# An attention and two feed-forward layers on one core: GpSimd takes the next weight slot's sums first, ScalarE splits weights a step sooner and the product first

## The reference

```python
kv  = einsum('bhsd,bhse->bhde', k, v)            # B=4, H=8, S=576, D=64
out = einsum('bhsd,bhde->bhse', q, kv)
x   = out / sqrt(mean(out**2, -1) + 1e-6) * g_norm    # then (2304, 512)
g   = x @ w_gate; val = x @ w_val                     # 512 -> 1536
x   = (g * sigmoid(g) * val) @ w_out                  # 1536 -> 512
h   = x @ w_in                                        # 512 -> 2048
y   = softplus(h) @ w_out2                            # 2048 -> 512
```

## Time and profile before

| what | value |
|---|---|
| median of 3 runs | 890.45 us |
| the profiled execution | 890.55 us, of it span 888.8 us |
| PE | busy 877.7 us, 99% of the span |
| PEld (weight loads) | 814.4 us, 92% |
| DVE | 645.2 us, 73% |
| ACT | 441.5 us, 50% |
| POOL | 229.7 us, 26% |
| granted clock of TensorE | 1.0 in all 40 slices |

### The profile page before, as it was taken

The page is one execution under the profiler, slowest core; times in us unless marked ns, Lnnn a source line. Parts: engine busy times, 40 slices in busy tenths (PEclk is TensorE's granted clock), DMA queues, the critical chain, the costliest instruction groups (busy, mean ns, idle before and its releaser), DMA issues.

```text
span 888.8 us, 14699 instructions
## 1 busy us (share of the span) xinstructions
PE 877.7 (99%) x5362; PEld 814.4 (92%) x5362; DVE 645.2 (73%) x1254; ACT 441.5 (50%) x778; POOL 229.7 (26%) x189
## 2 busy tenths in 40 slices
PE   8999999999899999999999999999999999999998
PEld 7999999999899999999999999999999999999997
DVE  3555665777575866676777998878878878878875
ACT  4617464664342544343345664554554554554553
POOL 4644203289820398730255000000000000000000
PEclk9999999999999999999999999999999999999999
DMA  9985865442200022010034110000000000000100
GB/s 270 227 213 151 154 139 127 126 114 72 72 1 1 1 72 68 22 44 1 1 96 129 62 48 0 36 0 0 35 0 0 35 0 0 35 0 0 37 1 36
DMA packets 95541, 53.93 MB, mean 61 GB/s; under 512 B 37248, under 2 KB 86528, under 8 KB 95488
## 3 DMA queue, kind: packets, MB, share of 16 engines
q1 hardware_dynamic: 95328, 53.23, 22.5%
q10 hardware_dynamic: 160, 0.00, 0.0%
HBM read 44.96 MB, written 8.26 MB: 60 GB/s over the span
## 4 chain that ended last, share of the span: by engine, by line
PE 88%; POOL 5%; DVE 2%; issue 2%; ACT 1%; DMA 1%; SPq 1%; DVEq 0%; ACTq 0%; POOLq 0%
PE bank L951 20%; PE bank L953 20%; PE bank L952 20%; PE bank L1110 7%; PE bank L1109 7%; PE bank L1108 7%; POOL slots L748 2%; PE bank L891 1%; PE bank L884 1%; POOL slots L751 1%; PE bank L959 1%; POOL slots L743 1%; DMA raw_out<-in_moe_w_out 0%; POOL slots_sums L734 0%; POOL slots_sums L732 0%
## 5 line engine op out<-in xcount | busy, mean ns | idle before, releaser
L951 PE MATMUL bank<-x_hi,arena 128*128 128x384 f32 x554 | 187.0, 338 | 0.0
L953 PE MATMUL bank<-x_hi,arena 128*128 128x384 f32 x554 | 186.8, 337 | 0.0
L952 PE MATMUL bank<-x_lo,arena 128*128 128x384 f32 x554 | 186.0, 336 | 0.0
L951 PE MATMUL bank<-ring,slots 128*128 128x256 f32 x504 | 143.1, 284 | 3.4 <-DVE sum_b L1595 2.5
L952 PE MATMUL bank<-ring,slots 128*128 128x256 f32 x504 | 142.6, 283 | 0.0
L953 PE MATMUL bank<-ring,slots 128*128 128x256 f32 x504 | 142.6, 283 | 0.0
L1333 ACT ACTIVATE act_a<-bank 128x384 f32<-128x384 f32 x96 | 47.2, 491 | 173.9 <-PE bank L953 173.9
L1110 PE MATMUL bank<-arena,g_lo 128*128 128x512 f32 x288 | 113.1, 393 | 0.0
L1109 PE MATMUL bank<-arena,g_hi 128*128 128x512 f32 x288 | 112.9, 392 | 0.0
L1108 PE MATMUL bank<-arena,g_hi 128*128 128x512 f32 x288 | 111.9, 388 | 0.0
L951 PEld LDWEIGHTS bank<-x_hi,arena 128*128 128x128 f32 x554 | 104.4, 188 | 4.0
(11 more groups left out here) (140 smaller groups left out, 1653.5 us busy)
## 6 DMA issues: line engine op xcount, KB each, us to landing
stage<-in_moe_w_out SPq DMA_DIRECT2D x28, 256.0 KB, 3.8
out_dram<-out_stage SPq DMA_DIRECT2D x18, 256.0 KB, 2.1
k<-in_k SPq DMA_DIRECT2D x16, 256.0 KB, 3.3
v<-in_v SPq DMA_DIRECT2D x16, 256.0 KB, 3.2
stage<-in_moe_w_in SPq DMA_DIRECT2D x16, 256.0 KB, 2.8
xy<-in_q SPq DMA_DIRECT2D x48, 72.0 KB, 3.0
stage<-in_moe_w_gate SPq DMA_DIRECT2D x12, 256.0 KB, 3.8
stage<-in_moe_w_val SPq DMA_DIRECT2D x12, 256.0 KB, 4.0
```

The lines of the kernel that those rows point to most:

```text
L951: nc.tensor.matmul(ps, hi, rhs_hi, start=first, stop=False)
L952: nc.tensor.matmul(ps, hi, rhs_lo, start=False, stop=False)
L953: return nc.tensor.matmul(ps, lo, rhs_hi, start=False, stop=last)
```

## The change

`weight_highs(f)` now also makes the output's high part, so that part comes ahead of the sums' high part in the counts of `w7_hi_ready`, and `HIGH7_AT` and `SUM_HIGH7_AT` put slots 0 to 2 one step sooner (slot 8's raw high one later). On POOL the sums' low part becomes a function of its own, and the next slot's sums stand ahead of it; the output's low part stands ahead of both, and `load7_out` waits only for that. SP issues the loads of slot 2 and the w_out of slot 1 two tiles sooner. On ACT `g7_high(q)` stands ahead of `weight_sum_highs`.

```diff
-LOWS7_RAW = 2
+LOWS7_RAW, LOWS7_OUT = 2, 3
...
-HIGH7_AT = {19: 0, 20: 1, 22: 2, 25: 3, 26: 4, 27: 5, 38: 6, 39: 7, 40: 8, 42: 9, 43: 10, 44: 11}
+HIGH7_AT = {18: 0, 19: 1, 21: 2, 24: 3, 25: 4, 26: 5, 38: 6, 39: 7, 41: 8, 42: 9, 43: 10, 44: 11}
-SUM_HIGH7_AT = {20: 0, 21: 1, 24: 2, 25: 3, 26: 4, 27: 5, 38: 6, 39: 7, 41: 8, 42: 9, 43: 10, 45: 11}
+SUM_HIGH7_AT = {19: 0, 20: 1, 22: 2, 24: 3, 25: 4, 26: 5, 38: 6, 39: 7, 41: 8, 42: 9, 43: 10, 45: 11}
...
         def load7_out(f):
...
-                sp.wait_ge(w7_ready, LOWS7 * f)
+                sp.wait_ge(w7_ready, LOWS7 * (f - 1) + LOWS7_OUT)
...
         load7_up(1)
-        for j in range(1, NT - 1):
+        keep_x(3, 1)
+        fetch_x(3, 1)
+        load7_up(2)
+        load7_out(1)
+        for j in range(2, NT):
             keep_x(3, j)
             fetch_x(3, j)
-        load7_up(2)
-        load7_out(1)
-        keep_x(3, NT - 1)
-        fetch_x(3, NT - 1)
...
             pool.wait_ge(w7_hi_ready, 3 * f + 2)
+            nc.gpsimd.tensor_tensor(slots7[:, f % SEG, RAW7 + OUT7:SLOT7], raw7_out[:, :],
+                                    slots7[:, f % SEG, OUT7:RAW7].bitcast(F32), ALU.subtract).then_inc(w7_ready, 1)
+
+        def weight_sum_lows(f):
+
+            pool.wait_ge(w7_hi_ready, 3 * f + 3)
             for i in (3, 5):
                 nc.gpsimd.tensor_tensor(w7_part(f, 1, i, i + 2), w7_sum(f, i, i + 2),
                                         w7_part(f, 0, i, i + 2).bitcast(F32), ALU.subtract).then_inc(w7_ready, 1)
-            pool.wait_ge(w7_hi_ready, 3 * f + 3)
-            nc.gpsimd.tensor_tensor(slots7[:, f % SEG, RAW7 + OUT7:SLOT7], raw7_out[:, :],
-                                    slots7[:, f % SEG, OUT7:RAW7].bitcast(F32), ALU.subtract).then_inc(w7_ready, 1)
...
-        for f in range(SEG):
+        weight_sums(0)
+        weight_lows(0)
+        weight_sums(1)
+        weight_sum_lows(0)
+        weight_lows(1)
+        weight_sum_lows(1)
+        weight_sums(2)
+        weight_lows(2)
+        first_x_sum(1)
+        for f in range(3, SEG):
             weight_sums(f)
+            weight_sum_lows(f - 1)
             weight_lows(f)
-            if f == 1:
-                first_x_sum(1)
+        weight_sum_lows(SEG - 1)
...
         def weight_highs(f):
...
+            act.wait_ge(raw7_out_loaded, 16 * (f + 1))
+            nc.scalar.activation(slots7[:, f % SEG, OUT7:RAW7], raw7_out[:, :], ACT.Copy).then_inc(w7_hi_ready, 1)
 
         def weight_sum_highs(f):
...
-            act.wait_ge(raw7_out_loaded, 16 * (f + 1))
-            nc.scalar.activation(slots7[:, f % SEG, OUT7:RAW7], raw7_out[:, :], ACT.Copy).then_inc(w7_hi_ready, 1)
...
+            g7_high(q)
             if k in SUM_HIGH7_AT:
                 weight_sum_highs(SUM_HIGH7_AT[k])
-            g7_high(q)
```

More of the change, by code:

```diff
@@ L794, in _ @@
         first_x_sum(3)
-        for f in range(SEG, NF1):
+        weight_sums(SEG)
+        weight_lows(SEG)
+        for f in range(SEG + 1, NF1):
             weight_sums(f)
+            weight_sum_lows(f - 1)
             weight_lows(f)
+        weight_sum_lows(NF1 - 1)
         x_sums(3)
```

## The result

The changed kernel is slower by 0.7%: 897.19 us, the median of 6 runs (895.88 to 898.24), against 890.58 us for the kernel before (6 runs, 889.33 to 892.93). The ratio is 1.0072, with a 95% interval of 1.0055 to 1.0088. The forecast was 897.7. The profiled execution took 896.48 us with a span of 894.7; before it was 890.55 with 888.8. On ACT, VectorE and TensorE the lines of the changed kernel have numbers 16 higher than before, apart from the weight work itself (L1231 is now L1247, L1236 is L1254, L1238 is L1249).

What follows compares the result with a forecast made beforehand. TensorE, busy 99% of the span, was taken as the bound, so only its idle time counts. 0.4 + 8.15 + 2.5 + 0.1 - 3.9 = +7.25 us on 890.55, less 0.1, gave 897.7 us; range 893.0 to 901.0.

Steps and rivals of the forecast that it cites:

- Slot 2: Step 21: ACT waits for a w_out load queued behind work its own root starts; cost 8.15 us, bounds 5 and 10.
- VectorE's slow instruction: Ring's low part beside POOL's sums' lows of slot 1 takes 2.48 us, not 0.83; root late by 1.7 us.
- The clock: Behind slot 2's wait the granted clock falls; 5 us slow, 2.5 us lost, bounds 0 and 3.5.
- Slot 1: Step 19: w_out lands at 176.4, so silu(20) ends after TensorE wants up1(21); cost 0.4 us, bounds 0 and 1.5.
- The later slots: From seven-product step 0: late w_out landings stay covered; three ACT instructions ahead of sum_a expose 0.1 us, up to 1.5.
- The gain: Five TensorE waits at new weight slots vanish through the product's earlier place and POOL's earlier sums; 3.9 us, bounds 0 and 4.3.
- Rival (c): Removed waits return as w_out waits in steps 2 to 5 and 15 to 20; 901.6 to 902.6 us, chance 5%.

Runs made afterwards that it cites:

- e2: Changed kernel plus 42 extra 128x384 products into an unneeded PSUM bank, ahead of TensorE's wait of step 23; 895.09 us, ratio 1.0044.
- e3: Kernel before, with only the product's high part put ahead of the sums' high part on ACT; 891.04 us, ratio 0.9999.
- e7: Changed kernel, SP order kept, with slot 2's output high part moved behind the SiLU of step 23 and its sums' high part with it; 893.38 us.
- e5: e4 with the product's high part put behind the sums' high part on ACT again; 886.14 us, ratio 0.9948.
- e4: Changed kernel with w_out loads issued sooner on SP: slot 2's behind fetch (3, 2), slot 1's ahead of fetch (3, 1); 886.41 us, ratio 0.9944.
- e6: e4 with ACT's early ring part put ahead of the sums' high part; 885.92 us, ratio 0.9954.

## Why the prediction was right, and where it was not

**Slot 2: the place and the mechanism right, the size a little high.** 8.15 us were forecast, 7.4 measured. The landing is 4.38, exactly as in the earlier trace rows. The root was 1.8 us later than in the earlier trace rows, against 1.7 in the working. What was too large is the way from root to fetch: 4.99 us in the working, 187.66 to 191.35 = 3.7 in the trace. It is the tile's store that was quicker: from its issue to the fetch 3.66 us before (187.16 to 190.82) and 2.35 here (189.00 to 191.35).

**VectorE's slow instruction.** The 1.7 rested on the ring's low part taking 2.48 us and not 0.83. VectorE and POOL at that time in the changed kernel:

```profile
182.71 2.45 DVE L1596 SCALAR_TENSOR_TENSOR ring<-xy,gain,ring 128x256 fp32r<-128x256 f32 x2
```

```profile
182.18 2.70 POOL L754 TENSOR_TENSOR slots<-slots_sums,slots 128x512 fp32r<-128x512 f32 x2 [3.60 <-ACT slots L1254]
```

2.45 us for the pair, beside a POOL instruction pair that covers nearly all of it. The Trainium skill, "SBUF — State Buffer", "Who interferes with whom", says that a VectorE instruction with two SBUF inputs contends with a GpSimd instruction that reads SBUF; the trace agrees, with 2.45 us here against 0.83 beside an idle POOL.

**The clock: right, and the length in part by luck.** 2.5 us forecast, 2.4 measured by the length of the step, 2.1 by e2. The working had assumed 5 us slow; it was from 199.73 to about 204.7. That figure was taken from the slow products at the start, where the granted clock reads 1.00 throughout, so nothing shows that those products were slow by the clock. Behind the stops of e3 and e7 the slow stretch was some 3.4 us and not 5. The fall came about 2 us after the last product and not 3, which changed nothing here; in e3 a rest of 1.97 us in all was enough for one. The Trainium skill's page "TensorE: Matmul & The Clock Gate", "The HAM clock gate", with its two levels and its fall after rest, was rightly counted against the change; the trace agrees, with 1.00 before the rest and 0.50 behind it.

**Slot 1: 0.4 forecast, 0.9 measured,** inside its bounds of 0 to 1.5. ACT's copy started at 175.88 and not 176.4, that is 0.5 us sooner than in the working. But TensorE was 0.7 us sooner in this execution (tile root 163.71, against 164.23 in the earlier trace rows, 0.5 of it), so it waited for longer. Part of the difference is thus this execution's start and not the change.

**The later slots: 0.1 forecast, 0.7 measured.** The working counted three ACT instructions ahead of `sum_a`, and not the ring part ahead of `sum_b` on VectorE, which took 1.42 us.

**The gain: the size right, the reason half wrong.** 3.9 us forecast, 4.2 measured with the overlap. But the prediction gave ACT's order as the cause ("Their cause is ACT's order") and counted the product's place as one of two remedies. e3 shows that the product's place alone gains nothing, and e5 that the waits stay away without it. The cause lies with POOL's sums, which come too late for ACT (9.3 us a slot against steps of 7.78); ACT's order only chose who waited. Which of POOL's order, the tables and the loads brought them forward is open.

**Rival (c), the removed waits coming back as waits on w_out: rightly excluded, for a reason that holds only in part.** At the later slots the cover was there, and more of it than the 1.4 us counted: ACT waits for w_out 0.23 to 2.77 us at slots 5, 7, 10 and 11, the four that the prediction named, the longest at 368.96, and TensorE does not wait. At slots 3 and 4 it was TensorE's own stop that left the loads time; e7 shows 4.38 us of exactly this wait at slot 4 where the stop is gone and slot 2 is late all the same.

The terms measured are 0.9 + 7.4 + 2.4 + 0.7 - 4.2 = +7.2 against +7.25 forecast. The sum came out closer than its parts: 0.85 too much for slot 2 and the clock stood against 1.1 too little for slot 1 and the later slots, and 0.3 more gain than forecast. The 5.9 us between the two profiled executions are less than 7.2 because of two things outside the prediction, the 0.7 before slot 1 and the 0.5 at 478.55. The medians differ by 6.6; which of the profile's terms is smaller in the other runs is not known.

## What to carry to other kernels

Before a wait is moved to an earlier place in an in-order engine, write down what stands behind it there, and follow what it waits for back through the DMA queue: if that chain passes through the same engine, the wait is as long as the chain less what the engine still does in the meantime (here 9.5 us from root to landing, of it 8.45 waited). Price a stop of TensorE as the wait plus the slow products behind it, and look at the granted clock even behind a stop of 2 us. And where a single-buffer chain of load, copy and free runs through several engines, mend the load's time first: moving the reader only moved the wait in e7, and putting the product ahead of it only handed it on in e3. The good half of this change with two w_out loads placed sooner (e4, e5, e6) runs in about 886 us, 0.5% under the kernel before.

## What was not expected of the hardware

- A rest of 7.4 us cost 2.4 us more: 15 products started 0.32 us apart in place of 0.17. The granted clock was already down to 0.64 on average in the window from 194 to 196, with the last product at 192.12. In e2, products whose result nobody reads kept it at 1.00, and the step behind them began 0.16 us later than without them.
- A rest of 1.97 us (e3) was followed by some 3.4 us at half clock as well, about 1.6 us lost, and one of 4.38 us (e7) by the same. In both the clock fell only after the products had begun again. The rests of 0.65 and 0.92 us in the kernel before left it at 1.00.
- The w_out load of 256 KB behind a fetch and two raw loads landed in 4.38 us in both kernels, where the median of seven such loads was 2.8.
- The wait of 0.71 us at 478.55 in before is 0.20 us in the changed kernel, in steps that the change does not touch. No run was made for it, and its cause stays open.
